# More TensorE work ahead of the first scores, and one tail copy moved ahead of the first inverse

## The chip, the cores and the metric

The kernel runs on one core of a Trainium2 chip. The metric is the device time of one execution in microseconds (us); lower is better. Engines are named as in the profile: PE is TensorE (PEld its weight loads), DVE VectorE, ACT ScalarE, POOL GpSimd, SP the engine that issues most DMAs.

## The reference, cut to what matters

Inputs: q, k, v of 4 batches x 8 heads x 576 positions x 64, float32. Three layers follow one another; the change is in the first.

```
rel    = pos[:, None] - pos[None, :]
scores = q @ k.T / sqrt(64) - slope[h] * |rel|,  kept where 0 <= rel < 128
attn   = softmax(scores) ;  x = attn @ v                      # 2304 tokens x 512
logits = x @ phi ; slots = softmax over tokens(logits).T @ x  # 32 slots
slot_out[e] = relu(slots[e] @ w1[e]) @ w2[e]                  # 8 experts, 1024 hidden
x = softmax over slots(logits) @ slot_out
out = (relu(x @ w_in) ** 2) @ w_out                           # 2048 hidden
```

## The kernel before

Five engine programs run side by side, with semaphores between them. The attention works on 16 pairs of heads, g = 0 to 15. Each engine calls its own `step(n)` for n = -2 to 17, and what stands in a step runs in exactly that order on that engine, so an instruction that waits holds up all behind it.

For one pair, in order of the data:

- SP loads q, k, the 64 tail positions of both (`tail_in`) and v. A transfer for a later pair waits until its buffer is free.
- POOL (for pair 0: DVE and ACT) puts two heads side by side in `q_in` and `k_in` (line L514, `order_pair`).
- PE transposes them into PSUM: `transpose_q` (L992), `transpose_k` (L1014), `transpose_tails` (L1000), each against the identity matrix `ident`. ACT copies out q (`take_q`, L849), DVE copies out k (`take_k`, L600) and the tails (`take_tails`, L591 and L594, which give `kT`'s last columns and `q_tailT`).
- PE makes the scores in two rounds (`scores(g, 0)` and `scores(g, 1)`, L1033) and the tail's (`tail_scores`, L1042). `scores(1, 0)` of the second pair waits for its q and k; `scores(1, 1)` waits in addition for `tail_taken` 3, that is for `take_tails(2)`.
- DVE masks each tile and finds its row's extreme (L562); ACT exponentiates it and sums the row (L831). ACT's order for pair 0 is: two tiles, then `take_q(1)`, then the other six tiles, then the tail.
- DVE inverts the row sums: `invert(g, 0)` for the eight tiles (L610, L613), `invert(g, 1)` for the tail. POOL multiplies the probabilities by them (`normalize`, L503 and L507).
- PE transposes the probabilities (L1059, L1063), ACT and DVE copy them out, PE makes the outputs (L1077, L1083).

PE's order in the first steps is: warm-up products, `transpose_q(0)`, `transpose_k(0)`, `transpose_tails(0)`, `scores(0, 0)`, `scores(0, 1)`, `transpose_q(1)`, `transpose_tails(1)`, `tail_scores(0)`, `transpose_k(1)`, `transpose_q(2)`, `transpose_tails(2)`, `scores(1, 0)`, `scores(1, 1)`, `tail_scores(1)`, `transpose_k(2)`, then the first pair's probabilities.

The warm-up products multiply `ident` by itself into PSUM bank 0, which the scores overwrite. They wait for `consts_ready` 3 (`ident` and `fold` written). One float32 product is two MATMUL instructions in the trace, one transpose is one:

```
pe.wait_ge(consts_ready, 3)
for _ in range(3):
    mm(psum[:, 0, 0:P], ident[:, :], ident[:, :], start=True, stop=True)
attention(step)
```

After the attention come the logits (L1126), the tokens in rows (L1137), the slots' inputs (L1175), the experts (L1227 and L1248, weights by DMA into a ring), `w_in` (loads issued at L447), and the last layer, 9 blocks of 256 tokens (L1300, L1319 to L1321).

Of the kernel before, what the change touches and what calls it, by code (L numbers as in the profile page):

```python
# [11 lines left out]
P = 128  # L12
# [53 lines left out]
def attention_moe_ffn(nc, q, k, v, phi, w1, w2, w_in, w_out, out):  # L66
# [11 lines left out]
    with ctx:  # L78
# [5 lines left out]
        def sb(name, shape, dt=F32):  # L84
            size = 4
            for n in shape[1:]:
                size *= n
            t = nc.alloc_sbuf_tensor_at(name, shape, dt, offset=place["at"])
            place["at"] += (size + 31) // 32 * 32
            assert place["at"] <= SBUF_TO, (name, place["at"])  # L90
            return t


        ident = sb("ident", [P, P])
# [105 lines left out]
        psum = ctx.enter_context(nc.psum_tensor("psum", [P, 8, 512], F32))  # L200
# [98 lines left out]
        def since(eng, s, value):  # L299

            if not isinstance(value, int) or value > 0:
                eng.wait_ge(s, value)

        NP = B * PAIRS
# [25 lines left out]
        def tail_in_bank(g):  # L330

            return (BK_O, BK_PT + 1)[g] if g < 2 else tail_bank(g - 2)
# [205 lines left out]
        def _(dve):  # L538
# [26 lines left out]
            def mask_round(g, r):  # L565
                par = g % 2
                for i in ROUNDS[r]:
                    c0, off = P if i == 0 else 0, 256 * (i % 2)
                    for h in range(2):
                        if i == ROUNDS[r][0]:  # L570
                            dve.wait_ge(s_done, 5 * g + 2 * r + h + 1)
                        if i == 0:
                            since(dve, pt_done, 4 * (g - 2) + 2 * h + 2)
                        masked_min(probs[:, par, h, i, c0:2 * P], psum[:, score_bank(g, r, h), off + c0:off + 2 * P],
                                   rel[:, c0:2 * P], SLOPES[2 * (g % PAIRS) + h], row_min[:, par, 4 * h + i:4 * h + i + 1])

            def mask_tail(g):
                par = g % 2
                dve.wait_ge(s_done, 5 * g + 5)
                if g == 0:  # L580
                    dve.wait_ge(rel_ready, 2)
                masked_min(probs_tail[:, par, 0:P + TAIL], psum[:, score_bank(g, 2, 0), 0:P + TAIL],
                           rel_tail[:, :], SLOPES[2 * (g % PAIRS)], row_min[:, par, 8:9])

            def take_tails(g):
                two = g % 2
                if g == 0:
                    dve.wait_ge(pads_ready, 1)
                dve.wait_ge(tail_done, g + 1)
                tail = psum[:, tail_in_bank(g), TAIL_T:TAIL_T + P]  # L590
                nc.vector.tensor_copy(kT[:, two, 4 * P:S], tail[:, TAIL:P])  # L591
                for h in range(2):
                    rows, to = slice(D * h, D * h + D), TAIL * h
                    last = nc.vector.tensor_scalar(q_tailT[rows, two, to:to + TAIL], tail[rows, 0:TAIL],  # L594
                                                   QSCALES[2 * (g % PAIRS)], None, ALU.mult)
                last.then_inc(tail_taken, 1)

            def take_k(g):
                dve.wait_ge(trk_done, g + 1)
                nc.vector.tensor_copy(kT[:, g % 2, 0:4 * P].rearrange("p (x t) -> p x t", t=4),  # L600
                                      psum[:, k_bank(g), :].rearrange("p (t x) -> p x t", t=4)).then_inc(trk_taken, 1)

            def take_probs(g, h):
                dve.wait_ge(pt_done, 4 * g + 2 * h + 2)
                nc.vector.tensor_copy(probsT[:, 2 + h, :], psum[:, BK_PT + 1, :]).then_inc(ptB_taken, 1)  # L605

            def invert(g, part):
                par, cols = g % 2, slice(0, 8) if part == 0 else slice(8, 9)
                dve.wait_ge(exp_done, 9 * g + 8 + part)
                nc.vector.tensor_scalar(sum_eps[:, par, cols], row_sum[:, par, cols], EPS, None,  # L610
                                        ALU.add).then_inc(eps_done, 1)
                dve.wait_ge(eps_done, 2 * g + part + 1)
                nc.vector.reciprocal(row_inv[:, par, cols], sum_eps[:, par, cols]).then_inc(inv_done, 1)  # L613
                if g == LAST and part == 0:
                    dve.wait_ge(inv_done, 2 * g + 1)
                    nc.vector.tensor_tensor(probs[:, par, 1, :, :], probs[:, par, 1, :, :],
                                            row_inv[:, par, 4:8].unsqueeze(2).to_broadcast([P, 4, 2 * P]),
                                            ALU.mult).then_inc(norm_last, 1)

            def step(n):  # L620
                if n == -2:
                    dve.wait_ge(q_raw_loaded[0], 16)
                    nc.vector.tensor_copy(q_in[:, :, :, :], q_raw[:, 0, :, :, :].rearrange("p h t d -> p t h d")
                                          ).then_inc(first_q_ready, 1)
                if n == -1:
                    take_k(0)
                    take_tails(0)
                if 0 <= n < NP:
                    mask_round(n, 0)
                if 1 <= n <= NP:  # L630
                    invert(n - 1, 1)
                if 0 <= n < NP:
                    mask_round(n, 1)
                    mask_tail(n)
                if 0 <= n < NP - 1:
                    take_k(n + 1)
                if n == 0:
                    take_tails(1)
                if 1 <= n <= NP:
                    take_probs(n - 1, 0)  # L640
                if 0 <= n < NP:
                    invert(n, 0)
                if 0 <= n < NP - 2:
                    take_tails(n + 2)
                if 1 <= n <= NP:
                    take_probs(n - 1, 1)

            attention(step)


# [327 lines left out]
        def _(pe):  # L978
            mm = nc.tensor.matmul

            def transpose_q(g):
                two = g % 2
                if g == 0:
                    pe.wait_ge(first_q_ready, 1)
                else:
                    pe.wait_ge(q_ready, g)
                if g <= 2:
                    since(pe, trq_taken, g)
                else:
                    pe.wait_ge(trk_taken, g)  # L990
                for t in range(4):
                    last = nc.tensor.transpose(psum[:, BK_TR, P * t:P * t + P], q_in[:, t, :, :].rearrange("p h d -> p (h d)"), ident[:, :])  # L992
                last.then_inc(trq_done, 1)

            def transpose_tails(g):
                two = g % 2
                pe.wait_ge(tail_loaded[two], 32 * (g // 2 + 1))
                since(pe, masked, 9 * (g - 2) + 4)
                since(pe, o_tail_taken, g - 3)
                nc.tensor.transpose(psum[:, tail_in_bank(g), TAIL_T:TAIL_T + P], tail_in[:, two, :, :].rearrange("p h d -> p (h d)"), ident[:, :]  # L1000
                                    ).then_inc(tail_done, 1)
# [86 lines left out]
            def step(n):  # L1088
                if n == -2:
                    transpose_q(0)  # L1090
                    transpose_k(0)
                    transpose_tails(0)
                if 0 <= n < NP:
                    scores(n, 0)
                    scores(n, 1)
                if n == 0:
                    transpose_q(1)
                    transpose_tails(1)
                if 0 <= n - 2 < NP:
                    outputs(n - 2)  # L1100
                if n == NP:
                    pe.wait_ge(phi_loaded, 16)
                    logits(0)
                    logits(1)
                if 0 <= n < NP:
                    tail_scores(n)
                if 0 <= n < NP - 1:
                    transpose_k(n + 1)
                if 0 <= n - 1 < NP:
                    transpose_probs(n - 1, 0)  # L1110
                if 0 <= n < NP - 2:
                    transpose_q(n + 2)
                    transpose_tails(n + 2)
                if 0 <= n - 1 < NP:
                    transpose_probs(n - 1, 1)
# [28 lines left out]
                    nc.tensor.transpose(psum[:, BK_WARM, 0:P], ident[:, :], ident[:, :])  # L1144

            pe.wait_ge(consts_ready, 3)
            for _ in range(3):
                mm(psum[:, 0, 0:P], ident[:, :], ident[:, :], start=True, stop=True)
            attention(step)
            logits(2)  # L1150
# [250 lines left out]
```

## Time and profile before

| what | value |
|---|---|
| median of 3 runs | 424.74 us (424.46 to 425.55) |
| the profiled execution | 423.91 us |
| its span, first to last instruction | 422.1 us |
| PE busy | 402.9 us, 95% of the span |
| DVE, ACT, POOL busy | 243.4, 218.8, 97.9 us |
| moved by DMA | 61.34 MB |

The profiled execution is one of its own, 0.83 us below the median of the timed ones. Of its 423.91 us, 1.8 lie outside the span. The profile puts every instruction at a time from the span's start; matmuls are pipelined, so the row of a group runs from the start of its first to the modelled end of its last, and groups of neighbours overlap.

### The profile page before, as it was taken

The numbers are of one execution on the slowest core, as the hardware profiler recorded it, in microseconds if no ns is written. First come the engines' busy times: TensorE is split into PE (matmuls) and PEld (weight loads), VectorE is DVE, ScalarE is ACT, GpSimd is POOL, SyncE is SP. The second block draws the span as 40 slices with busy tenths as digits, with TensorE's granted clock in tenths as the row PEclk, the third lists the DMA queues.
The fourth block names the chain that finished last, engine by engine and source line by source line (L and its number), as shares of the span: only waits on it lengthen the run. The fifth ranks groups of instructions, "written<-read, shape, count | busy, mean of one in ns | idle before, by whom it ended". The sixth has DMA issues, their size and how long they took to land.

```text
span 422.1 us, 7944 instructions
## 1 busy us (share of the span) xinstructions
PE 402.9 (95%) x2873; PEld 310.1 (73%) x2873; DVE 243.4 (58%) x680; ACT 218.8 (52%) x560; POOL 97.9 (23%) x94
## 2 busy tenths in 40 slices
PE   6699999999989999989899999999999999999996
PEld 5588888888777554333688888888888888888884
DVE  4788888888855543113999545454545445454520
ACT  3889898989854311003965444444443434444420
POOL 4578787878650010000142000000000000000000
PEclk9999999999999999999999999999999999999999
DMA  6689898997725799999600101010101001010101
GB/s 183 160 238 291 246 309 257 289 269 237 201 79 178 251 371 398 405 383 386 222 2 0 51 0 51 0 50 2 50 2 50 0 0 50 0 50 2 50 0 50
DMA packets 49858, 61.34 MB, mean 145 GB/s; under 512 B 25504, under 2 KB 33696, under 8 KB 48288
## 3 DMA queue, kind: packets, MB, share of 16 engines
q1 hardware_dynamic: 49280, 60.37, 42.7%
q10 hardware_dynamic: 544, 0.52, 0.4%
q8 instruction: 21, 0.34, 0.3%
q14 instruction: 13, 0.11, 0.1%
HBM read 56.16 MB, written 4.72 MB: 144 GB/s over the span
## 4 chain that ended last, share of the span: by engine, by line
PE 84%; ACT 5%; DMA 4%; DVE 4%; SPq 1%; issue 1%; POOL 0%; ACTq 0%; POOLq 0%
PE psum L1319 15%; PE psum L1320 15%; PE psum L1321 15%; PE psum L1033 6%; PE psum L1077 6%; PE psum L1059 5%; PE psum L1300 4%; DMA win_sb<-in_moe_w_in 3%; PE psum L1227 3%; ACT probs L831 3%; PE psum L992 2%; PE psum L1248 2%; PE psum L1137 2%; PE psum L1042 2%; PE psum L1014 2%; SPq L447 1%
## 5 line engine op out<-in xcount | busy, mean ns | idle before, releaser
L1319 PE MATMUL psum<-wout_hi,act_hi 128*128 128x512 f32 x288 | 113.2, 393 | 1.8 <-DVE wout_lo L755 1.5
L1320 PE MATMUL psum<-wout_lo,act_hi 128*128 128x512 f32 x288 | 112.9, 392 | 0.0
L1321 PE MATMUL psum<-wout_hi,act_lo 128*128 128x512 f32 x288 | 112.1, 389 | 0.0
L781 DVE TENSOR_TENSOR sq_h<-relu_h 128x512 f32<-128x512 f32 x72 | 56.3, 782 | 78.4 <-ACT relu_h L940 78.3
L940 ACT ACTIVATE relu_h<-psum 128x512 f32<-128x512 f32 x72 | 43.1, 599 | 92.0 <-PE psum L1300 86.1
L831 ACT ACTIVATE probs<-probs,row_min 128x256 f32<-128x256 f32 (+1 forms) x128 | 60.1, 471 | 13.5 <-DVE row_min L562 13.5
L503 POOL TENSOR_TENSOR probs<-probs,row_inv 128x1024 f32<-128x1024 f32 x31 | 59.2, 1928 | 23.2 <-DVE row_inv L613 23.2
L1321 PEld LDWEIGHTS psum<-wout_hi,act_lo 128*128 128x128 f32 x288 | 54.1, 188 | 11.8
L1319 PEld LDWEIGHTS psum<-wout_hi,act_hi 128*128 128x128 f32 x288 | 54.1, 188 | 11.8 <-issue 1.9
L1320 PEld LDWEIGHTS psum<-wout_lo,act_hi 128*128 128x128 f32 x288 | 54.3, 189 | 8.7
L785 DVE TENSOR_TENSOR act_lo<-sq_h,act_hi 128x512 fp32r<-128x512 f32 x72 | 49.8, 692 | 5.4 <-ACT act_hi L943 0.6
L943 ACT ACTIVATE act_hi<-relu_h 128x512 fp32r<-128x512 f32 x72 | 45.6, 634 | 4.7 <-ACT relu_h L940 0.6
L562 DVE CUSTOM_DVE_ANT_0 probs<-psum,rel 128x256 f32<-128x256 f32 (+1 forms) x128 | 42.1, 385 | 4.1 <-PE psum L1033 4.0
L1033 PE MATMUL psum<-kT,qT 64*128 64x256 f32 (+1 forms) x256 | 30.5, 378 | 2.9 <-DVE q_tailT L594 1.9
L1059 PE MATMUL psum<-ident,probs 128*128 128x128 f32 x224 | 30.3, 274 | 2.4 <-ACT probsT L845 1.4
L1300 PEld LDWEIGHTS psum<-combT,mix 128*128 128x128 f32 x144 | 26.7, 188 | 7.0 <-issue 1.8
L1300 PE MATMUL psum<-combT,mix 128*128 128x256 f32 (+1 forms) x144 | 29.1, 286 | 0.0
L605 DVE COPY probsT<-psum 128x512 f32<-128x512 f32 x32 | 22.1, 691 | 10.9 <-PE psum L1063 10.8
L1077 PE MATMUL psum<-probsT,v_in 128*64 128x256 f32 (+1 forms) x256 | 27.7, 359 | 0.6 <-ACT probsT L845 0.6
L1059 PEld LDWEIGHTS psum<-ident,probs 128*128 128x128 f32 x224 | 25.2, 141 | 3.6 <-issue 2.0
L1033 PEld LDWEIGHTS psum<-kT,qT 64*128 64x128 f32 x256 | 21.9, 195 | 7.7 <-issue 2.7
L1077 PEld LDWEIGHTS psum<-probsT,v_in 128*64 128x64 f32 x256 | 17.3, 136 | 12.3 <-issue 5.6
(143 smaller groups left out, 436.1 us busy)
## 6 DMA issues: line engine op xcount, KB each, us to landing
ring<-in_moe_w SPq DMA_DIRECT2D x16, 1024.0 KB, 6.2
ring<-in_moe_w SPq DMA_DIRECT2D x4, 2048.0 KB, 13.6
out_x<-out_sb SPq DMA_DIRECT2D x9, 512.0 KB, 2.8
q_raw<-in_q SPq DMA_DIRECT2D x16, 256.0 KB, 3.6
v_in<-in_v SPq DMA_DIRECT2D x32, 128.0 KB, 2.6
ring_late<-in_moe_w SPq DMA_DIRECT2D x2, 2048.0 KB, 9.4
ring_x<-in_moe_w SPq DMA_DIRECT2D x2, 2048.0 KB, 8.0
win_sb<-in_moe_w_in SPq DMA_DIRECT2D x4, 1024.0 KB, 14.4
```

Of the source, the lines that this page charges most:

```text
L503: nc.gpsimd.tensor_tensor(probs[:, par, h, 0:4, :], probs[:, par, h, 0:4, :], row_inv[:, par, 4 * h:4 * h + 4].unsqueeze(2).to_broadcast([ ...
L781: nc.vector.tensor_tensor(sq_h[:, u % 2, :], relu_h[:, u % 2, :], relu_h[:, u % 2, :], ALU.mult).then_inc(sq_done, 1)
L785: nc.vector.tensor_tensor(act_lo[:, 2 * u:2 * u + 2, :], sq_h[:, u % 2, :].rearrange("p (c t) -> p c t", c=2), act_hi[:, 2 * u:2 * u + 2, ...
L831: nc.scalar.activation(t, t, ACT.Exp, bias=row_min[:, par, one:one + 1], scale=-1.0, accum_out=row_sum[:, par, one:one + 1]).then_inc(exp_ ...
L943: nc.scalar.activation(act_hi[:, 2 * u:2 * u + 2, :], relu_h[:, u % 2, :].rearrange("p (c t) -> p c t", c=2), ACT.Square).then_inc(hi_done, 1)
L1033: last = mm(psum[:, score_bank(g, r, h), off + c0:off + 2 * P], qT[rows, two, P * i:P * i + P], kT[rows, two, P * (i - 1) + c0:P * (i + 1) ...
L1059: last = nc.tensor.transpose(psum[:, BK_PT + half, at:at + P], probs[:, par, h, i, c:c + P], ident[:, :])
L1077: mm(psum[D * h:D * h + D, BK_O, P * j:P * j + w], v_in[:, two, h, j, :], probsT[:, 2 * a[0] + h, a[1]:a[1] + w], start=(j == 0), stop=(j ...
L1300: last = mm(psum[:, u % 4, FT * x:FT * x + FT], mix[:, P * (2 * u + x):P * (2 * u + x) + P], cols, start=True, stop=True)
L1319: mm(to, hi, wout_hi[:, c, :], start=first_of, stop=False)
L1320: mm(to, hi, wout_lo[:, c, :], start=False, stop=False)
L1321: last = mm(to, lo, wout_hi[:, c, :], start=False, stop=last_of)
```

## The change

Three edits. PE makes six warm-up products instead of three. PE makes six transposes of `ident`, which nothing reads, behind `transpose_tails(0)` and ahead of `scores(0, 0)`, into the same bank 0. DVE does `take_tails(2)` ahead of `invert(0, 0)` instead of behind it; in later steps the order stays.

```
@@ DVE, step(n)
                     take_tails(1)
                 if 1 <= n <= NP:
                     take_probs(n - 1, 0)
+                if n == 0:
+                    take_tails(2)
                 if 0 <= n < NP:
                     invert(n, 0)
-                if 0 <= n < NP - 2:
+                if 1 <= n < NP - 2:
                     take_tails(n + 2)
                 if 1 <= n <= NP:
                     take_probs(n - 1, 1)
@@ PE, step(n)
                     transpose_q(0)
                     transpose_k(0)
                     transpose_tails(0)
+                    for _ in range(6):
+                        nc.tensor.transpose(psum[:, 0, 0:P], ident[:, :], ident[:, :])
                 if 0 <= n < NP:
                     scores(n, 0)
                     scores(n, 1)
@@ PE, ahead of attention(step)
             pe.wait_ge(consts_ready, 3)
-            for _ in range(3):
+            for _ in range(6):
                 mm(psum[:, 0, 0:P], ident[:, :], ident[:, :], start=True, stop=True)
             attention(step)
```

## Rows read from the trace of the kernel before

**Rows 1.** Busy time by stretch: us, PE, PEld, DVE, ACT, POOL (instructions), PEclk, DMA, GB/s

```profile
12.00:14.00 2.00, 1.85 (x13) 1.59 (x12) 1.63 (x8) 1.76 (x6) 1.17 (x2) 1.00 0.72 239
...
22.00:115.00 93.00, 92.64 (x882) 75.14 (x882) 78.14 (x368) 83.65 (x301) 69.66 (x64) 1.00 0.86 262
...
152.00:178.00 26.00, 25.98 (x330) 11.45 (x330) 8.87 (x21) 3.31 (x8) 0.30 (x1) 1.00 1.01 390
```

**Rows 2.** Chain that ended last, 12 to 25 us: start, length, what

```profile
12.24 0.69 ACT qT L849
12.92 2.95 ACT probs L831 x12
...
16.10 0.20 DVE row_inv L613
...
20.10 0.52 POOL probs_tail L507
...
20.66 0.55 PE psum L1059 x3
...
22.85 1.72 PE psum L1033 x16
```

**Rows 3.** Timeline of PE, 2 to 18 us: start, length, instructions, idle before and releaser

```profile
2.23 1.65 PE L1148 MATMUL psum<-ident 128*128 128x128 f32 x6 [2.23 <-DVE fold L549]
4.94 1.12 PE L992 MATMUL psum<-ident,q_in 128*128 128x128 f32 x4 [1.07 <-DVE q_in L623]
5.85 1.06 PE L1014 MATMUL psum<-ident,k_in 128*128 128x128 f32 x4
6.70 0.42 PE L1000 MATMUL psum<-ident,tail_in 128*128 128x128 f32 x1
7.79 3.36 PE L1033 MATMUL psum<-kT,qT 64*128 64x128 f32 x16 [0.66 <-DVE kT L600]
11.08 1.12 PE L992 MATMUL psum<-ident,q_in 128*128 128x128 f32 x4
...
12.20 0.67 PE L1042 MATMUL psum<-kT,q_tailT 128*128 128x192 f32 x2
12.71 0.60 PE L1014 MATMUL psum<-ident,k_in 128*128 128x128 f32 x4
13.14 0.60 PE L992 MATMUL psum<-ident,q_in 128*128 128x128 f32 x4
...
16.98 1.13 PE L1033 MATMUL psum<-kT,qT 64*128 64x256 f32 x8 [1.91 <-DVE q_tailT L594]
```

**Rows 4.** Timeline of DVE, 9 to 17 us

```profile
9.44 0.29 DVE L562 CUSTOM_DVE_ANT_0 probs<-psum,rel 128x128 f32<-128x128 f32 x1 [1.30 <-PE psum L1033]
...
11.15 0.42 DVE L562 CUSTOM_DVE_ANT_0 probs<-psum,rel 128x256 f32<-128x256 f32 x1 [0.51 <-PE psum L1033]
...
12.91 0.36 DVE L562 CUSTOM_DVE_ANT_0 probs_tail<-psum,rel_tail 128x192 f32<-128x192 f32 x1 [0.30 <-PE psum L1042]
...
14.08 0.45 DVE L594 TENSOR_SCALAR q_tailT<-psum 64x64 f32<-64x64 f32 x2
15.90 0.17 DVE L610 TENSOR_SCALAR sum_eps<-row_sum 128x8 f32<-128x8 f32 x1 [1.37 <-ACT probs L831]
...
16.48 0.45 DVE L594 TENSOR_SCALAR q_tailT<-psum 64x64 f32<-64x64 f32 x2
```

**Rows 5.** Timeline of ACT, its first exponential

```profile
9.78 0.40 ACT L831 ACTIVATE probs<-probs,row_min 128x128 f32<-128x128 f32 x1 [2.99 <-DVE row_min L562]
```

**Rows 6.** Timeline of POOL, 12 to 21 us

```profile
12.33 0.61 POOL L514 COPY q_in<-q_raw 128x512 f32<-128x512 f32 x1 [4.11 <-PE psum L992]
...
16.39 3.75 POOL L503 TENSOR_TENSOR probs<-probs,row_inv 128x1024 f32<-128x1024 f32 x2 [2.34 <-DVE row_inv L613]
```

**Rows 7.** Line L382, the issue at 7.8 us: duration, start, time to landing

```profile
L382 SPq DMA_DIRECT2D tail_in<-in_k x1: 609/609/609, 7.8 to 7.8; - x1
...
DMA to landing us min/median/max: 2.3/2.3/2.3
```

More of the change, by code:

```diff
@@ L640, in step @@
                     take_probs(n - 1, 0)
+                if n == 0:
+                    take_tails(2)
                 if 0 <= n < NP:
                     invert(n, 0)
-                if 0 <= n < NP - 2:
+                if 1 <= n < NP - 2:
                     take_tails(n + 2)
@@ L1092, in step @@
                     transpose_tails(0)
+                    for _ in range(6):
+                        nc.tensor.transpose(psum[:, 0, 0:P], ident[:, :], ident[:, :])
                 if 0 <= n < NP:
@@ L1146, in _ @@
             pe.wait_ge(consts_ready, 3)
-            for _ in range(3):
+            for _ in range(6):
                 mm(psum[:, 0, 0:P], ident[:, :], ident[:, :], start=True, stop=True)
```

## The prediction

> **What bounds the kernel now.** I read the busy time by stretch first, to see where the change can matter at all. From 22 to 115 us PE is busy 92.64 of 93 us, so there the attention runs at PE's own pace and a change can only shift it [rows 1]. The three edits lie ahead of that stretch. The second view is the chain that ended last, in order of time: what does the steady stretch wait for? Behind PE's first scores (7.79) and the second pair's q transposes (11.08) [rows 3] it goes through ACT (`take_q(1)` at 12.24, then the exponentials that stand behind it), DVE (inverse at 16.10), POOL (normalization, to 20.62) and back to PE at 20.66; from 22.85 it is PE alone [rows 2]. The reader is to see that PE's own 1.91 us of idle time at 15.07 is not on this chain [rows 3]: PE would otherwise only reach the wait for POOL sooner.
>
> The third view is PE's timeline. Four transposes of 128x128 start 0.85 us ahead of the next group at 5.85 (5.85 to 6.70, 213 ns each), but 0.43 us at 12.71 (12.71 to 13.14, 108 ns each) [rows 3]. That is TensorE at 1.2 GHz until about 12.2 and at 2.4 GHz from 12.7 at the latest, although the granted clock reads 1.00 in that stretch as everywhere else [rows 1]; I trust the durations. The same doubling is in the scores: 16 instructions take from 7.79 to 11.08 at the low level and 1.72 us at 22.85 [rows 2, 3]. Ahead of the rise PE had worked without a pause since 7.79; ahead of that it had paused 1.07 us behind the warm-up and 0.66 us ahead of the scores [rows 3]. These are the two holes that the change fills.
>
> **Edit 1, three more products.** Six more instructions. The six at 2.23 end at 3.88; less one instruction's 0.42 tail and plus one slot they hold PE until about 3.67 [rows 3]. Six more slots of 0.213 us are 1.28, so the next work could start at 4.95, where `transpose_q(0)` starts at 4.94. By the mean pace of the first six, (1.65 - 0.42) / 5 = 0.245, it would be 5.11 to 5.15. Cost 0 to 0.2 us; I take 0.1. Cover: the wait for `q_in` on DVE. Once that is gone, each product costs its 0.43.
>
> **Edit 2, six transposes.** At the low level 6 x 0.213 = 1.28 us from 6.91 (6.70 plus a slot), to 8.19, where the scores start at 7.79: 0.40 us late, and with edit 1's worst 0.6. At the high level 6 x 0.108 = 0.65, to 7.56, and hidden in the 0.66 us wait for DVE's `kT` copy [rows 3]. So this edit is free or costs 0.4, by when the clock rises.
>
> **What both buy.** In the new kernel PE works without a pause from 2.23, 5.56 us earlier than from 7.79. I place the rise as much earlier: 12.2 to 12.7 less 5.56, 6.6 to 7.2. The late bound: the products of the warm-up don't help, and only the work from 4.94 on counts as the start; the rise then comes 7.79 - 4.94 = 2.85 earlier, 9.4 to 9.8. Beyond it is no earlier rise at all (a rival). The early bound is a rise before the first transposes, which I price by their slots: k and tails ready up to about 0.4 sooner.
>
> With the rise near 7 the scores start at 7.79 + 0.1, take 1.72 and not about 3.3, the four transposes behind them 0.43 and not 0.91 (1.12 less the 0.21 by which a low-level matmul's end lies behind its slot), and the last one's tail 0.16 and not 0.21. `transpose_q(1)` is then done at 7.89 + 1.72 + 0.43 + 0.16 = 10.20, and `take_q(1)` on ACT starts there, 2.0 us ahead of 12.24 [rows 2, 3]. Is ACT free? DVE's first mask is 1.65 us behind the start of the scores now [rows 3, 4], about 0.9 at the high level; ACT's first exponential is 0.34 behind that [rows 4, 5], and two tiles take it 0.9. That is 7.89 + 0.9 + 0.34 + 0.9 = 10.0: just free. Behind `take_q(1)` ACT is fed faster than it works (it took 12.92 to 15.87 for 12 pieces on end [rows 2]), so the exponentials end 2.0 us sooner, at 13.87.
>
> With the late rise, at 9.6, the scores start at 8.19, and of the 4.2 us of low-level slots to the last transpose (7.79 to 11.08, and 0.91) 1.4 are done at the low level and 2.8 in 1.4: done by 11.0 + 0.2, gain 1.0. With the early bound the gain is 2.4 to 2.5.
>
> **Edit 3, the tails.** No instruction is added. `take_tails(2)` takes about 0.6 us (from the inverse's end at 16.30 [rows 2] to 16.93 [rows 4]). Now DVE must have it done ahead of the inverse at 13.87. From the tail's mask to the end of `take_tails(1)` is 12.91 to 14.53, 1.62 us [rows 4]; the eight masks before that took 12.91 - 9.44 = 3.47 with 0.81 of waits for PE in it [rows 4], so 2.7 from 8.8, and the tail's mask can start at 11.5, `take_tails(1)` ends at 13.1 and the moved copy at 13.7: 0.2 us before the inverse is due. Queued behind it on DVE are the inverse, and through it POOL and PE. Its own wait is for `transpose_tails(2)`, behind `transpose_q(2)`, which needs POOL's `q_in`: that copy is released by `transpose_q(1)`, not by its transfer (4.11 us of idle time end with PE [rows 6]), so it moves to about 10.3 and ends at 10.9. The tails' last transfer is issued at 7.81 and lands 2.3 later, at 10.1 [rows 7]. Transposed by 11.6, they are in time. What the edit gives: `scores(1, 1)` starts sooner (the 1.91 us), and the second pair's masks 0.6 sooner. Neither sets the chain: PE waits for POOL at 20.66 anyway. I take 0, bounds -0.3 to +0.2.
>
> **Sum.** The inverse comes 2.0 us sooner, POOL's 3.75 + 0.5 us follow unchanged [rows 2, 6], PE's steady stretch starts at about 18.6 and not 20.66. Later transfers hang on PE's progress: from 152 to 178 us the DMAs are full (a share of 1.01 [rows 1]), but their issues wait for buffers that PE frees, so they shift along. For the profiled execution 423.91 - 2.0 = 421.9 us; it lies 0.83 below the median, so for the median 424.74 - 2.0 = **422.7 us**.
>
> **A rule that speaks against it.** The Trainium skill, "TensorE: Matmul & The Clock Gate", Part 4, says that transposes don't bring TensorE's clock up as products do. The trace of before doesn't decide it, since its rise at about 12.4 follows 3.3 us of products and 1 us of transposes. By that rule the filled hole at 6.91 is filled with nothing that counts, which is the first rival. The same page, Part 1, says that the rise can come at a different point of the same kernel from run to run; one trace can't show it.
>
> **Rivals.**
>
> *Only products raise the clock* (0.17). Then the products from 2.23 to 4.95 are too short a piece (the scores' own 3.3 us were needed now), the clock stays low to the end of the scores and rises as late as before; the six transposes cost 0.40 and edit 1 up to 0.17: 424.74 + 0.5 = 425.2 us. For it: the rise came right behind the scores' products. Against: twice as many warm-up products are nearly as long as the scores.
>
> *The gain is lost later* (0.12): the shifted attention meets the full DMA stretch [rows 1] with some transfer that doesn't shift: 424.7. Against: each issue there waits for PE.
>
> *The moved tails hold the inverse* (0.08). They were transposed at 13.84 before (13.14 + 0.43 + 0.27 [rows 3]). If they come no sooner, DVE copies them to 14.45 and the inverse is 1.4 sooner than 15.90 and not 2.0: 423.4. It decides once the tails are transposed after 13.3, 0.6 ahead of 13.87.
>
> *The clock falls again, on the other side* (0.06). With the early work done faster PE is idle more between 11 and 18.6; now it was idle 1.91 us there [rows 3], and the level stayed. If it falls there, the steady stretch starts at the low level and gives up half its time until the next rise. The piece before the rise took 7.79 to 12.5, 4.7 us, now, giving up 2.4: 425.1. Measured from 2.23 it took 10.3, giving up 5.1: 427.8. It is a loss from 4.0 us of low level in the steady stretch on.
>
> **How the numbers follow.** The forecast has 0.57, with its own range from 422.1 (early bound) to 423.8 (late rise). The whole range reaches to the first rival: 421.8 (the early bound, and 0.3 for the spread of the runs of before) to 425.3, which leaves out the fall of the clock alone. A measurement of this kernel tells 0.3%, 1.3 us, from no change. Faster by more: the forecast without its late rises, 0.52, and half of the held inverse, 0.04: 0.56. Within: the first rival, the lost gain, the late rises and the rest, 0.36. Slower by more: 0.08, the fall of the clock and what else I don't see.
>
> **What would show it.** In the profile after, the transposes L1014 of the first pair or the unread ones at about 108 ns apart, the 16 scores of the first pair in 1.7 us from 7.9, `take_q(1)` at 10.2, the inverse's first part at 13.9, POOL's L503 at 14.4, PE's steady stretch from 18.6. `scores(1, 1)` no longer waits for `q_tailT` behind the inverse. I am wrong if the scores take 3.3 us from 8.2 (first rival), if the inverse waits for DVE's own tails, if L1014 or L992 are back at 213 ns apart between 12 and 22, or if the steady stretch starts 2 us sooner and the time stays.

## The result, and the profile after

The changed kernel takes 421.8 us (median of 12 executions, 421.21 to 425.34) against 424.81 us of the kernel before on the same chip (12 executions, 423.65 to 426.8): a ratio of 0.9942, 95% interval 0.9918 to 0.9967, or 2.5 us less (1.4 to 3.5). The two medians are 3.0 apart, which lies inside that interval. The forecast was 422.7, 2.0 us less, with a range of 421.8 to 425.3.

The profiled execution of the changed kernel took 423.65 us, only 0.26 less than that of before. So the two traces can't be compared by their ends; they have to be compared stage by stage. First the chain that ended last, as in [rows 2]; its columns are start, length, what:

```profile
7.31 1.79 PE psum L1035 x16
9.10 0.60 PE psum L994 x4
...
9.72 0.69 ACT qT L851
10.41 2.95 ACT probs L833 x12
...
13.59 0.22 DVE row_inv L613
...
17.59 0.52 POOL probs_tail L507
...
18.15 0.55 PE psum L1061 x3
...
20.34 1.72 PE psum L1035 x16
```

The links shown are those of [rows 2], and each behind the scores is 2.5 us sooner: `take_q(1)` at 9.72 (12.24), POOL's last multiplication at 17.59 (20.10), PE's return at 18.15 (20.66), the third pair's scores at 20.34 (22.85). (Between the inverse and POOL's last multiplication the profile leads the chain of before another way, through `take_tails(2)` at 16.34 and the second pair's masks; but POOL was busy there too, with the 3.75 us from 16.39 of [rows 6].) What PE did differently adds up to it: the scores start 0.48 sooner, take 1.79 and not 3.36 us, 1.57 less, and the transposes behind them 0.60 and not 1.06, 0.46 less, 2.5 in all. PE's timeline, with the instructions of [rows 3], shows since when:

```profile
2.23 2.93 PE L1152 MATMUL psum<-ident 128*128 128x128 f32 x12 [2.23 <-DVE fold L549]
4.95 1.04 PE L994 MATMUL psum<-ident,q_in 128*128 128x128 f32 x4
5.81 0.63 PE L1016 MATMUL psum<-ident,k_in 128*128 128x128 f32 x4
6.27 0.27 PE L1002 MATMUL psum<-ident,tail_in 128*128 128x128 f32 x1
6.38 0.82 PE L1096 MATMUL psum<-ident 128*128 128x128 f32 x6
7.31 1.79 PE L1035 MATMUL psum<-kT,qT 64*128 64x128 f32 x16
...
15.08 0.59 PE L1044 MATMUL psum<-kT,q_tailT 128*128 128x192 f32 x2 [1.08 <-DVE row_min L562]
```

The four q transposes start 0.86 us ahead of the k transposes (1.2 GHz), the k transposes 0.46 ahead of the tail's (2.4 GHz). The level rose near 5.9 us; in the trace of before near 12.5 [rows 3]. The six unread transposes ran at the high level, 6.38 to 7.20, inside the wait for the `kT` copy.

DVE's timeline shows the end of the moved copy and the first inverse:

```profile
12.36 0.45 DVE L594 TENSOR_SCALAR q_tailT<-psum 64x64 f32<-64x64 f32 x2
13.39 0.17 DVE L610 TENSOR_SCALAR sum_eps<-row_sum 128x8 f32<-128x8 f32 x1 [0.58 <-ACT probs L833]
```

Where did the 2.5 us go by the end? They are all there when the experts begin (L1231 at 149.97, before 152.47). Then comes the wait for the last expert's first weights. Busy time by stretch around it, in the columns us, PE (instructions), PEclk, DMA, GB/s:

```profile
176.00:179.90 3.90, 0.00 (x0) 1.00 1.00 382
179.90:183.30 3.40, 3.38 (x32) 0.50 1.05 389
183.30:186.00 2.70, 2.70 (x25) 0.99 1.05 387
```

and the same place on PE's timeline, after, and then before:

```profile
179.92 3.60 PE L1231 MATMUL psum<-ring,siT 128*32 128x256 f32 x32 [4.01 <-DMA ring<-in_moe_w]
```

```profile
181.46 1.93 PE L1227 MATMUL psum<-ring,siT 128*32 128x256 f32 x32 [3.04 <-DMA ring<-in_moe_w]
```

The weights landed 1.54 sooner and not 2.5. And after 4.01 us without work the granted clock fell to 0.50 and the expert's 32 products took 3.60 and not 1.93 us: 1.67 lost. The rest differs by little: from the start of these products to the first of L1323 it is 23.03 us (L1319 before: 21.75, with 0.31 of wait for `w_in`), and from there to the start of PE's last instruction 214.53 in both. So 1.54 sooner and 1.28 longer leave the 0.26 us between the two executions.

So one fact about the executions is needed to read all that follows. Each is listed with its mean granted clock, which tells whether the clock fell anywhere behind its first rise (the trace counts the time ahead of the first rise as 1.00). Of the traces' falls, those that leave a mean of 0.998 or more stand behind PE's last instruction (e10: from about 420.2 us) and cost nothing. Of the changed kernel's 12 executions, 7 have a mean clock of 1.0 and lie at 421.21 to 421.86; 5 have 0.992 to 0.996 and lie at 422.84 to 425.34. The kernel before, in the 79 executions beside the experiments: 13 at 0.998 or more with a median of 423.7 us, 66 below with 425.11. Falls are common in both, and rarer in the changed kernel (5 of 12 against 66 of 79, from different batches of executions).

### The profile page after: what moved, and what is told of

The parts are those of the page before. It is cut to its first block, busy times and chain, and to the rows that moved or that the text cites. A ratio compares the mean times of both kernels' runs of the same rounds, so it can differ in the third digit from the quotient of the medians.

```text
span 421.9 us, 7968 instructions
## 1 busy us (share of the span) xinstructions
PE 403.5 (96%) x2885; PEld 310.4 (74%) x2885; DVE 243.2 (58%) x680; ACT 218.8 (52%) x560; POOL 97.9 (23%) x94
## 4 chain that ended last, share of the span: by engine, by line
PE 85%; ACT 5%; DMA 4%; DVE 3%; issue 1%; POOL 1%; POOLq 0%; ACTq 0%
PE psum L1323 15%; PE psum L1324 15%; PE psum L1325 15%; PE psum L1035 6%; PE psum L1079 6%; PE psum L1061 5%; DMA ring<-in_moe_w 4%; PE psum L1304 4%; PE psum L1231 3%; ACT probs L833 3%; PE psum L994 2%; PE psum L1252 2%; PE psum L1141 2%; PE psum L1044 1%; PE psum L1016 1%
## 5 line engine op out<-in xcount | busy, mean ns | idle before, releaser
L1323 PE MATMUL psum<-wout_hi,act_hi 128*128 128x512 f32 x288 | 113.2, 393 | 1.8 <-DVE wout_lo L757 1.5
L1325 PEld LDWEIGHTS psum<-wout_hi,act_lo 128*128 128x128 f32 x288 | 54.1, 188 | 11.8
L1323 PEld LDWEIGHTS psum<-wout_hi,act_hi 128*128 128x128 f32 x288 | 54.1, 188 | 11.8 <-issue 1.9
L1035 PE MATMUL psum<-kT,qT 64*128 64x256 f32 (+1 forms) x256 | 28.9, 363 | 0.8 <-issue 0.5
L1035 PEld LDWEIGHTS psum<-kT,qT 64*128 64x128 f32 x256 | 20.8, 187 | 5.2 <-issue 3.2
## 6 DMA issues: line engine op xcount, KB each, us to landing
ring<-in_moe_w SPq DMA_DIRECT2D x4, 2048.0 KB, 13.7
```

Source lines behind the costliest of these rows:

```text
L1035: last = mm(psum[:, score_bank(g, r, h), off + c0:off + 2 * P], qT[rows, two, P * i:P * i + P], kT[rows, two, P * (i - 1) + c0:P * (i + 1) ...
L1323: mm(to, hi, wout_hi[:, c, :], start=first_of, stop=False)
L1325: last = mm(to, lo, wout_hi[:, c, :], start=False, stop=last_of)
```

## The experiments

All are compared with the kernel before. "Falls" counts executions with a mean granted clock under 0.998.

**e1: only the products.** `transpose_q(0)` follows six products, the pause ahead of the scores stays.

```
-            for _ in range(3):
+            for _ in range(6):
                 mm(psum[:, 0, 0:P], ident[:, :], ident[:, :], start=True, stop=True)
```

> Only the six warm-up products, no unread transposes, DVE as before. Theory (clock, first hole): in the changed kernel TensorE reached its high level at about 5.85 us, before the second hole is even reached, so filling the first hole alone brings the rise. Then the scores start near 7.3, take 1.8 us and not 3.3, PE's steady stretch starts 2.3 to 2.5 us sooner than at 22.85, and the time is 421.8 to 422.3 us. Rival (second hole): the work must run without a pause into the scores; with the pause ahead of the scores left, the rise comes behind them, at 10 to 12.5, and the time is 424 to 425.

422.94 us, ratio 0.9956 (0.9930 to 0.9983), 7 falls of 12. Its trace shows an execution with a late rise and with falls, on PE's timeline:

```profile
7.73 3.36 PE L1033 MATMUL psum<-kT,qT 64*128 64x128 f32 x16 [0.66 <-DVE kT L600]
11.02 0.90 PE L992 MATMUL psum<-ident,q_in 128*128 128x128 f32 x4
...
16.71 1.13 PE L1033 MATMUL psum<-kT,qT 64*128 64x256 f32 x8 [2.16 <-DVE q_tailT L594]
```

and by stretch (us, PE, PEclk, DMA, GB/s):

```profile
18.40:21.80 3.40, 3.26 (x16) 0.50 0.28 84
```

The scores still ran at the low level, the rise came among the transposes at 11.02, and behind the 2.16 us wait the clock fell again, from 18.4 to 21.8 (and once more at the last expert). That execution took 425.92 us. But the five executions without a fall lie at 421.0 to 422.5, where a rise behind the scores would have left them near 423.7. That points to a rise that comes early in some executions and late in others of one kernel. The trace of e10, below, has the same start as e1 and shows the early case: its scores take 1.79 us. So the first hole alone brings the rise early at least in part.

**e2: only the unread transposes**, six of them behind `transpose_tails(0)`, three warm-up products.

```
                     transpose_tails(0)
+                    for _ in range(6):
+                        nc.tensor.transpose(psum[:, 0, 0:P], ident[:, :], ident[:, :])
```

> Only the six unread transposes, warm-up of three products and DVE as before. Theory (clock, first hole): the pause from 3.88 to 4.94 us stays, PE then works without one from 4.94, and the rise comes between 8.3 and 12; the transposes cost up to 0.4 us at the low level. Time 423.5 to 425.2. Rival (second hole is the one that counts): the rise is at or ahead of 8 us and the time is near 422.

424.95 us, ratio 1.0003 (0.9981 to 1.0026), 12 falls of 12. In its trace the six took 6.88 to 8.25, nearly all at the low level, so the scores started at 8.25, 0.5 late; they ran at the high level, so the rise came near 8.2:

```profile
6.88 1.44 PE L1094 MATMUL psum<-ident 128*128 128x128 f32 x6
8.25 1.79 PE L1033 MATMUL psum<-kT,qT 64*128 64x128 f32 x16
```

The gain of that was gone by the third pair, which starts at 22.8 as before: PE waited 1.73 us for `q_tailT` and worked at 0.50 from about 15.0 to 21.8. So in this execution the six transposes alone did bring the rise some 4 us earlier, and a fall took it back; no run has them alone with the later waits filled, which would tell what they are worth by themselves.

**e3: only DVE's order.**

```
+                if n == 0:
+                    take_tails(2)
                 if 0 <= n < NP:
                     invert(n, 0)
-                if 0 <= n < NP - 2:
+                if 1 <= n < NP - 2:
                     take_tails(n + 2)
```

> Only DVE's order, PE as before. Theory: the copy is done in DVE's wait for the exponentials, the first inverse stays at 15.90 us, POOL's first multiplication at 16.39, scores(1, 1) of PE start 1.9 us sooner and PE waits that much longer for POOL: 424.8, within 0.3 us. Rival: the 1.91 us of PE's wait was on the path, 423.0.

424.76 us, ratio 1.0006 (0.9979 to 1.0034). POOL's first multiplication started at 16.25. PE's waits moved: 1.49 us ahead of 17.45 and 1.60 for POOL ahead of 20.51, 3.09 in all, where before had 1.91 and 0.98. That is what the theory said. Over all executions the edit alone moves no time that can be measured, which with this interval means less than about 1.2 us: its five executions without a fall lie at 422.61 to 423.01, those of before in the same batch (six) at 422.63 to 424.08.

**e4: both PE edits, DVE's order as before.**

> Both PE edits, DVE's order as before. Theory: the clock alone makes the gain; the second pair's masks are up to 0.6 us later but hidden behind POOL; same time as the changed kernel, 421.8 (421.3 to 422.3 where the clock stays high throughout). Rival: with the faster PE the order on DVE becomes the bound and 0.5 us are lost: 422.3.

423.38 us, ratio 0.9958 (0.9931 to 0.9984), 7 falls of 12; the changed kernel's ratio is 0.9942 (0.9918 to 0.9967). The intervals overlap, so the medians don't tell the two apart. Executions without a fall are the same (421.29, the changed kernel's 421.55). Its trace has the fall in the thin stretch, by stretch (us, PE, PEclk, DMA, GB/s):

```profile
11.00:14.50 3.50, 1.94 (x16) 1.00 0.74 203
14.50:18.00 3.50, 2.81 (x10) 0.51 0.79 202
18.00:21.40 3.40, 3.40 (x18) 0.50 0.39 111
```

and on PE's timeline:

```profile
15.19 2.08 PE L1033 MATMUL psum<-kT,qT 64*128 64x256 f32 x8 [1.72 <-DVE q_tailT L594]
```

The scores were done early (8.04 to 9.76), and yet the third pair started at 22.47, 1.2 us behind the 21.29 of a trace (e12, below) whose scores started 0.25 later and whose clock did not fall: 1.4 us given up. Against e11, which has DVE's order in common with e4 (scores at 8.37, third pair at 21.64), it is 1.2.

**e5 to e7: keep PE busy in the waits behind.** e5 adds unread transposes in the second pair's waits, e6 ahead of the wait for the last expert's weights (which now stands behind the wait for `hid_ready`), e7 has both. All three hold the whole change.

```
# e5, e7                                     # e6, e7: expert_in(e)
 if n == 1:                                   if e >= 2:
     fill(8)      # transposes of ident           pe.wait_ge(hid_ready, e - 1)
 tail_scores(n)                               if e == E - 1:
...                                               keep_warm(24)
 if g == 0 and h == 0 and half == 1:          wait_item(i)
     fill(12)
 if half == 1:
     pe.wait_ge(normB_done, g + 1)
```

> The changed kernel, with unread transposes also in the second pair's waits: 8 ahead of tail_scores(1), 12 ahead of the first wait for the tail's normalization. Theory (the clock falls in the thin stretch from 11 to 22 us in part of the executions, and costs there): no fall ahead of 22 us in the trace, fewer executions with a mean granted clock under 0.998 than the changed kernel's 5 of 12, those left from the expert's wait; median 421.6. Rival (the falls hang on nothing that PE does there): the share of executions under 0.998 is as before and the time is 421.8 to 422.5.

423.82 us, ratio 0.9967 (0.9944 to 0.9990), 9 falls of 12; the trace's is at the expert's wait (4.24 us without work, then 3.58 us for 32 products), none ahead of 22 us. The theory wanted fewer falls than 5 of 12 and a median of 421.6, and missed both: this place alone doesn't cure them. Six of the nine have a mean clock of 0.994 or 0.996, as an execution with one fall at the expert has; three, at 0.990, have more.

> The changed kernel, with 24 unread transposes (2.6 us at the high level) ahead of the wait for the last expert's first weights, where PE idled 4.01 us and the clock fell for 3.4 us. Theory: the clock no longer falls there, the last expert's 32 products take 1.9 us and not 3.6, and nearly all executions are at 421.3 to 421.9. Rival (DMA): the wait for the weights sets the time of the stage and the low clock was hidden; the median stays at 421.8 and the slower executions too.

422.27 us, ratio 0.9950 (0.9924 to 0.9976), 4 falls of 12, those at 424.1 to 425.2. In the trace the wait still lasts 1.62 us behind the fill, and the products take 1.93.

> Both fills in the changed kernel. Theory: the two places are the only ones where the clock falls, so nearly all of 12 executions have a mean clock of 1.0 and the median is 421.4 (421.0 to 421.9). Rival: falls elsewhere or a late first rise leave part of the executions above 422.5.

421.68 us (6 executions, 421.44 to 422.03), ratio 0.9926 (0.9903 to 0.9949), no fall. The trace by stretch, and PE at the expert's wait:

```profile
12.00:22.00 10.00, 9.51 (x79) 1.00 0.78 209
176.00:180.00 4.00, 3.12 (x36) 1.00 0.98 377
```

```profile
179.49 1.93 PE L1241 MATMUL psum<-ring,siT 128*32 128x256 f32 x32 [0.88 <-DMA ring<-in_moe_w]
```

**e8: does a transpose count?** The changed kernel with 12 unread transposes for its six warm-up products.

```
-            for _ in range(6):
-                mm(psum[:, 0, 0:P], ident[:, :], ident[:, :], start=True, stop=True)
+            for _ in range(12):
+                nc.tensor.transpose(psum[:, 0, 0:P], ident[:, :], ident[:, :])
```

> The changed kernel, with its six warm-up products (12 instructions) replaced by 12 unread transposes of the same size. Theory (any work without a pause raises the clock): the rise comes as in the changed kernel, between 5.5 and 9 us, and the time is 421.8. Rival (the rule that transposes don't count): nothing but transposes runs until the scores at 8.2, so the rise comes at 11 to 13 us and the time is 424.5 to 425.3.

423.13 us (10 executions), ratio 0.9961 (0.9933 to 0.9988), 6 falls of 10. PE's timeline, with nothing but transposes ahead of 7.21:

```profile
2.23 2.82 PE L1152 MATMUL psum<-ident 128*128 128x128 f32 x12 [2.23 <-DVE fold L549]
4.84 1.05 PE L994 MATMUL psum<-ident,q_in 128*128 128x128 f32 x4
5.70 0.64 PE L1016 MATMUL psum<-ident,k_in 128*128 128x128 f32 x4
6.17 0.28 PE L1002 MATMUL psum<-ident,tail_in 128*128 128x128 f32 x1
7.21 1.79 PE L1035 MATMUL psum<-kT,qT 64*128 64x128 f32 x16
```

The q transposes are 0.86 us long in slots, the k transposes 0.47: the clock rose near 5.8 with no product before it. That settles the first rival. The time is between the two expectations, in part because of the falls; the four executions without one are at 420.93, 421.00, 422.84 and 423.18, and what sets the last two apart isn't known.

**e9 to e12: the parts again, with the falls filled.** The fills stand in all four, so that what is left is the start. e9 is the kernel before with fills (14 transposes ahead of `scores(1, 1)`, 4 ahead of `tail_scores(1)`, 8 ahead of the tail's normalization, 24 at the expert), e10 the same with six products, e11 adds the six unread transposes (DVE's order as before, 12 and not 8 at the normalization), e12 is e7 again.

```
# e9, e10, e11: in scores(g, 1)
+                    if g == 1:
+                        fill(14)
                     if g >= 1:
                         pe.wait_ge(tail_taken, min(g + 2, NP))
```

> The kernel before, unchanged in its start (three products, pauses ahead of the transposes and the scores, DVE's order), with fills in the waits behind: 14 unread transposes ahead of scores(1, 1), 4 ahead of tail_scores(1), 8 ahead of the first wait for the tail's normalization, 24 ahead of the last expert's weights. Theory (the change's gain is two things, an earlier first rise worth 2.0 us and fewer later falls): the falls go, the rise stays at 11 to 13, and nearly all executions are where those of before with a mean clock of 1.0 are, 423.6 (423.0 to 424.1); against the changed kernel with both fills 1.9 to 2.0 more. Rival (all of the gain is falls avoided): 421.7.

> e9 with six warm-up products, so the first pause filled and the one ahead of the scores left. Theory (the pause ahead of the scores decides in part of the executions whether the rise comes ahead of the scores or behind them, as at 11.57 in e1's trace): a spread from 421.4 to 423.7, median between, 422.5. Rival (the first hole alone suffices): all at 421.4 to 421.9.

> Both PE edits and the fills of e9, DVE's order as before. Theory (DVE's new order is worth nothing on the path and only shortens PE's pause, which the fill does as well): 421.7, within 0.3 of the changed kernel with both fills. Rival (DVE's order sets the second pair): 422.2 or more. A third way: a rise behind 8 us makes the 14 transposes slow and late, up to 1.3 us in such executions.

> The changed kernel with both fills once more, beside e9 to e11 on the same chip, for more executions than the first six. Theory: mean clock 1.0 in nearly all, median 421.7 (421.4 to 422.0). Rival: the first six were luck, and about 4 of 10 are above 422.5, as for the changed kernel.

| kernel | median us, executions | ratio to before (95%) | falls |
|---|---|---|---|
| e9: before + fills | 423.87, 12 | 0.9969 (0.9951 to 0.9988) | 2 |
| e10: + six products | 421.23, 6 | 0.9903 (0.9876 to 0.9930) | 0 |
| e11: + six transposes | 422.24, 6 | 0.9926 (0.9898 to 0.9953) | 0 |
| e12: e7 again | 422.08, 6 | 0.9919 (0.9890 to 0.9948) | 0 |

e9 bears its theory out (423.6 expected): with the start of before, the fills alone give 1.3 us, and the rival, that all of the change's gain is falls avoided (421.7), is refuted. From e9 to e10 is the largest step, 0.9903 / 0.9969 = 0.9934, or 2.8 us, for three products; 2.3 if e9's two falls are left out. e10 contradicts the expected spread: five of its six lie at 420.4 to 421.7, and the sixth, 422.93, is the profiled one, which had its rise ahead of the scores. From e10 on, the transposes and DVE's order add no gain. e12's expectation (421.4 to 422.0) was missed: no execution has a fall, and yet three of six lie above 422.5. The traces of e11 and e12 have a late rise, ahead of 8.4 us; that the rise alone makes the spread isn't shown, since e10's slowest execution had it earlier. What the transposes can cost shows when the rise is late: in e12's trace,

```profile
6.87 1.49 PE L1102 MATMUL psum<-ident 128*128 128x128 f32 x6
8.29 1.83 PE L1039 MATMUL psum<-kT,qT 64*128 64x128 f32 x16
```

and in e10's, which has none,

```profile
7.74 1.79 PE L1039 MATMUL psum<-kT,qT 64*128 64x128 f32 x16 [0.66 <-DVE kT L600]
```

The best medians are e10's, and e7's and e12's together (12 executions, 421.68, no fall). e10's whole interval, up to 0.9930, lies below the changed kernel's ratio of 0.9942, but not below the latter's interval, so that it beats the changed kernel is not shown.

**All fourteen profiled executions side by side**, from their timelines: start of the first instruction of the third pair's scores (the steady stretch; the chain's piece begins up to 0.07 later), start of the last expert's first products, and the difference. In e10, e11 and e12 the profiled execution is the slowest of the six.

| | third pair | last expert | difference |
|---|---|---|---|
| before | 22.78 | 181.46 | 158.7 |
| e3 | 22.64 | 180.88 | 158.2 |
| e9 | 22.22 | 180.94 | 158.7 |
| e2 | 22.80 | 181.23 | 158.4 |
| e1 | 23.06 | 182.16 | 159.1 |
| e4 | 22.47 | 181.01 | 158.5 |
| e11 | 21.64 | 181.08 | 159.4 |
| e12 | 21.29 | 181.34 | 160.1 |
| e10 | 20.70 | 180.87 | 160.2 |
| e6 | 20.66 | 180.54 | 159.9 |
| e5 | 20.47 | 180.36 | 159.9 |
| e7 | 20.36 | 179.49 | 159.1 |
| after | 20.27 | 179.92 | 159.7 |
| e8 | 20.16 | 179.76 | 159.6 |

The first six average 158.6, the last eight 159.7: where the start was early, 1.1 us of it were missing when the last expert's weights had landed (e1, with a late start and 159.1, is level with e7). Between the two, PE's progress shifts fully (the experts begin 129.7 us behind the third pair in both traces of before and after); the load of the last expert's first weights is issued as much sooner, at 162.09 and not 164.60, but took 17.8 us to land and not 16.8.

## Why the prediction was right, point by point

- *The clock's rise is the lever.* Right (e1, and e10 against e9), and larger than forecast in this trace: near 5.9 and not 6.6 to 7.2, so that the k transposes ran fast too. That is the early bound, priced at 2.4 to 2.5, and the steady stretch came 2.5 sooner. In other executions the rise was later: 8.2 to 8.4 in the traces of e2, e11 and e12, inside my 6.6 to 9.8, and 11 to 11.8 in e1's.
- *Edit 1, 0 to 0.2 us.* The q transposes start at 4.95, as before, but in this execution `q_in` was ready at 4.6 and not 4.9, so up to 0.3 were spent, and won back. The edit alone gains: 1.9 us in e1, 2.8 in e10 against e9, as much as the whole change.
- *Edit 2, free or 0.4 us.* Free in the trace after; 0.55 late in e12's (8.29 against 7.74). I credited the rise to both edits together. Beside edit 1 the transposes add no time that can be measured (e11 isn't faster than e10); alone they brought the rise to 8.2 in e2's trace, but e2 gains nothing, as the clock fell behind it. Whether they make the early rise more frequent stays open: e1's one late rise speaks for it, e10's six executions against.
- *Edit 3, 0, bounds -0.3 to +0.2.* Right on the path: e3 is at 1.0006, and e11 without it is level with e12. The copy was done at 12.8 (forecast 13.7), and DVE waited 0.58 for ACT: it held nothing. Its use could be that it cuts PE's wait of 1.7 to 2.2 us (e1, e2, e4, each with a fall in that stretch) into waits of 0.50, 1.08 and 1.60. None of the traces with the new order falls there; before's, with the old order and 1.91 us, doesn't either. The lists of executions speak for it more than the traces. A mean clock of 0.992 or less, more than 6 us at the low level, have 11 of the 46 executions with the new order and an unfilled thin stretch (after 1 of 12, e3 4 of 12, e6 4 of 12, e8 2 of 10) and 77 of the 115 with the old one (before 52 of 79, e1 6 of 12, e2 12 of 12, e4 7 of 12). So it is likely that the edit cuts such time; it doesn't end them (e6), and since the batches differ and the mean doesn't say where the clock fell, it isn't shown.
- *The sum, 2.0 us.* Measured 2.5 (1.4 to 3.5). That the number came out as near as this is in part luck, and the median of 421.8 stands at the very edge of my range. Two terms were missing and partly cancel. The start gave up to 2.5, of which about 1 was not there when the last weights landed. And the medians hold falls of the clock, which I counted only as a danger of the change: they were already in 66 of 79 executions of before and in 5 of 12 after. The forecast carried a profiled execution without a fall over to a median that is mostly of executions with one. Without falls the two kernels are at 421.55 (7 executions) and 423.7 (13, of other batches): 2.1 apart, which is more than the 1.5 that the traces leave behind the last weights (2.5 less 1.0); the difference isn't explained.
- *Rivals.* Only products count: refuted by e8. The trace thus disagrees with the Trainium skill, "TensorE: Matmul & The Clock Gate", Part 4, which says that transposes don't bring the clock up as products do; the rise came near 5.8 us, for the float32 transposes used here. The Trainium skill, same page, Part 1, says that the rise falls at another point from run to run, and the traces agree: after, e5, e6, e7 and e12 do the same work up to the scores, and by the spacing of their instructions it comes near 5.9, 6.3, 6.6, 6.1 and 8.4. The clock falls again: real, in e1, e2 and e4, at the place named; e4 gave up 1.2 to 1.4 us of the start, less than the 2.4 I had priced. In the changed kernel falls are rarer than before. Gain lost later: in part, about 1 us and not all, at the full DMA stretch that I named; I held that every issue shifts, which is so, but the landings don't shift as much. The inverse held by the tails: no.

Why the last weights land relatively later after an earlier start is open. In all eight early traces the difference is 159.1 or more, in five of the other six 158.7 or less. From the issue of that load to its landing the DMAs moved 403 GB/s in both before (164.60 to 181.40) and after (162.09 to 179.90), so they were not slower: for 1.0 us more they moved something else. No experiment separates the loads, and one profile for each kernel isn't a measure of chance.

## What to carry to other kernels

Ahead of the first real work, fill the wait behind TensorE's first instructions; three products in a 1.1 us hole gave 1.9 to 2.8 us here (e1, and e10 against e9), because the whole first pair hung on scores at half speed. Filling the next hole as well gave nothing more that could be measured. Read the clock from the pace of equal instructions, not from the granted clock, ahead of its first rise. And look behind the start for waits like those of 1.7 to 4.2 us here: the clock fell at them in some executions and not in others, so count executions by their mean clock before comparing medians, and fill all such waits or expect no full cure (e5 alone and e6 alone left 9 and 4 falls of 12; both together, in e7 and e12, none in 12).

## What the runs showed of the hardware that was not expected

- Transposes alone raised TensorE's clock, near 5.8 us after a start at 2.23 (e8).
- The clock fell at the last expert behind or within waits of 2.79 to 4.24 us (e2 2.79, e4 2.89, e1 3.46, e8 3.95, after 4.01, e5 4.24), but not with 3.04 (before) or 2.60 (e3) and not with 1.90 or less. In e2 and e4 it fell about 1 us after work had begun again, so a wait's length alone doesn't tell. One fall over the whole of the expert's 32 products costs 1.67 us.
- Executions of one kernel differ by up to 4 us, and the slow ones are those with falls: 421.2 to 421.9 without and 422.8 to 425.3 with, for the changed kernel. Not all of the spread is falls: e12's six, without any, lie at 421.0 to 423.4.
